# Three edits and a new step order in a fused attention, Fourier mixing and MLP kernel on one core

## The chip, the core and the metric

The kernel runs on one core of a Trainium2 chip. The metric is device time in microseconds for one launch. All inputs and the output lie in HBM; scratch tensors for intermediate tokens and for prepared weights lie there too.

## The reference

Chunked attention with memory keys feeds a Fourier mixing block with an MLP, and a gated convolutional MLP follows.

```python
# attention: batch 4, 8 heads, 768 tokens, head size 64; chunks of 32 queries
# look at 16 keys to the left, 8 to the right, and 8 memory keys
scores = scale * np.matmul(q_c, k_full.transpose(0, 1, 3, 2))
a = softmax(scores);  out[:, :, c_start:c_end] = np.matmul(a, v_full)
...
X = np.fft.fft(np.fft.fft(x, axis=1), axis=2)      # x: (4, 768, 512)
u = x + np.real(X)
un = (u - mu) / np.sqrt(var + 1e-06)
x = u + np.maximum(un @ w_ch1, 0.0) @ w_ch2        # 512 -> 2048 -> 512
...
h = np.maximum(x @ w_in, 0.0)                      # 512 -> 1024
gate = sigmoid(conv over 3 tokens of h)
return (h * gate) @ w_out                          # 1024 -> 512
```

## The kernel before

Every matrix product of the Fourier and MLP parts is made from three products of numbers split in a high and a low part (float32r): low by high, high by low, high by high. So each operand is prepared in two steps: ScalarE (ACT) copies the raw value into the high part, which rounds it, and VectorE (DVE) subtracts that from the raw value and writes the low part.

**Stage 1** handles attention and Fourier mixing, batch by batch (b = 0 to 3), in tiles of 128 tokens (t = 0 to 5). Its steps are named and put in order by hand in the table `ORDER`, one list for each of TensorE (PE), ACT, DVE and GpSimd (POOL); each engine takes its steps strictly in this order, and semaphores keep the data right. The steps on PE are `scores` (L507, q by the key window), `turn` (L517, transposes of the probabilities), `values` (L534), `seq` (L543, eight per batch, the transform over tokens), `dim` (L543, two per batch, the transform over channels) and `mix` (L599, transposes back). On ACT: `exp`, `keep` (copy of turned probabilities, L360), `split` (high part of folded tokens, L367), `bh` (L374), `qs` (L382), `mirror`. On DVE: `shift` (L421, L426), `norm` (L435 to L446), `bl` (L452), `cm` (L462, L463), `mk` (L473, L474, adds x and the mixed result). On POOL: `fold` (L315 to L321) and `lower` (L329, low part of folded tokens). `seq` of b needs the folded and lowered tokens; its first run also needs the table over tokens (`seq_tab`), the first `dim` the table over channels (`dim_tab`). Both tables come from HBM as ready high and low parts, issued by POOL's steps `tabs` and `tabd`, in the middle of the loads of q, k and v, which the DMA queue of SyncE (SP) issues in a ring of three tiles.

**Stage 2** is the first MLP, for each batch in two groups of four pairs. A pair n expands tokens by two 128-column blocks of `w_ch1` in seven products of six matmuls (L975, a Strassen-like scheme: seven weight blocks, of which three are loaded ones, called A11, A12, A22 and one, S1, is loaded and then changed, and S2, S3, S4 are sums). The preparation of a pair is: `load_raw1` (SP, two loads, L712 and L714), `sums` (POOL, four adds, L758 to L764), `weights1` (ACT L771 for all seven high parts, DVE L813 for all seven low parts), and `store_w1` (POOL's queue, L725), which keeps the finished pair in HBM for later batches. The weights lie in a ring of three buffers, so pair 3 takes the buffer of pair 0 and waits for its products and its store. Results of a pair pass through `keep_first` (ACT, L801), `combine` and `complete` (DVE, seven adds L890, and four low parts L894) and `rectify` (ACT, L806). After four pairs comes `contract` (L995), eight weight tiles loaded by `load_raw2` (SP, L721). For the first batch the banks of the contraction are those in which the pair's results stood, so token tile 3 of its first weight tile waits until `complete(3)` has made all its adds.

The first pairs are worked into stage 1 by steps called `mlp`: on PE `mlp0` to `mlp2` turn normalised tokens, `mlp3` and `mlp4` are pair 0 and `mlp5` and `mlp6` pair 1. SP puts the stores of the last batch's tokens (`store_u`, L268) between the load of pair 2 and that of pair 3.

**Stage 3** is the gated convolution (L1327, L1337).

Of the kernel before, what the change touches and what calls it, by code (L numbers as in the profile page):

```python
# [1599 lines left out]
```

## Time and profile before

| | us |
|---|---|
| median of 3 runs | 993.39 |
| lowest and highest | 991.74, 995.04 |
| the profiled execution, its time | 991.06 |
| the profiled execution, its span | 989.3 |
| PE busy | 943.7 |
| DVE busy | 624.9 |
| ACT busy | 346.7 |
| POOL busy | 221.1 |

The rows below are times from the start of the span. In a row of a timeline the first number is the start, the second the duration; the bracket at the end tells how long the engine had been idle and what ended the wait. L975 is line 975 of the kernel before.

### The profile page before, as it was taken

The page shows a single profiled execution, that of the slowest core. Times are in us where ns is not written, and L with a number is a line of the kernel's source. Part 1 is how long each engine was busy: PE and PEld are TensorE (multiplying, and loading weights), DVE is VectorE, ACT ScalarE, POOL GpSimd, SP SyncE. Part 2 cuts the span into 40 slices and gives each one's busy share as a digit, 9 for nine tenths or more (in the row PEclk, how much of TensorE's full clock was granted, in tenths as well). Part 3 has the DMA queues.
Part 4 walks back from the last instruction along what each step waited for, and adds up shares of the span by engine and source line. Part 5 has one row for each costly group of instructions (what it writes and reads, how often), then busy time and mean ns, then how long its engine had stood idle before and what let it go on. Part 6 is the DMA issues. An engine that isn't in the chain of part 4 may idle for free.

```text
span 989.3 us, 15359 instructions
## 1 busy us (share of the span) xinstructions
PE 943.7 (95%) x6168; PEld 850.1 (86%) x6168; DVE 624.9 (63%) x1034; ACT 346.7 (35%) x583; POOL 221.1 (22%) x231
## 2 busy tenths in 40 slices
PE   5899997859999999999999999999999999999998
PEld 4788786858897998989989889898898898998997
DVE  5467759658586773776827767266486295393590
ACT  2444555314244231332312323124253254253341
POOL 5757758114020000000000000000024033042041
PEclk9999999889999999999999999999999999999999
DMA  9956733567435672544824536355120300301001
GB/s 336 356 178 235 277 120 108 217 230 283 184 142 231 215 260 67 195 147 155 308 79 161 181 117 233 129 160 179 60 70 1 128 1 22 106 0 42 22 1 64
DMA packets 50033, 148.41 MB, mean 150 GB/s; under 512 B 7856, under 2 KB 12080, under 8 KB 45616
## 3 DMA queue, kind: packets, MB, share of 16 engines
q1 hardware_dynamic: 44640, 85.16, 25.0%
q0 software_dynamic: 5184, 62.27, 16.8%
q8 instruction: 46, 0.75, 0.3%
q14 instruction: 19, 0.16, 0.0%
q10 hardware_dynamic: 144, 0.07, 0.0%
HBM read 115.50 MB, written 31.98 MB: 149 GB/s over the span
## 4 chain that ended last, share of the span: by engine, by line
PE 85%; DVE 5%; DMA 4%; POOL 3%; issue 1%; SPq 1%; ACT 1%; DVEq 0%; POOLq 0%; ACTq 0%
PE ps L995 25%; PE ps L975 22%; PE ps L1327 13%; PE ps L1337 13%; PE ps L543 5%; DMA k_win<-in_k 2%; PE ps L507 2%; DMA w_raw<-in_moe_w 1%; PE ps L1310 1%; PE ps L534 1%; PE ps L936 1%; DVE h_raw L890 1%; DVE w L813 1%; PE ps L517 1%; DVE h L894 1%
## 5 line engine op out<-in xcount | busy, mean ns | idle before, releaser
L995 PE MATMUL ps<-w,h 128*128 128x512 f32 x1152 | 267.3, 391 | 0.4 <-DVE h_raw L890 0.4
L995 PEld LDWEIGHTS ps<-w,h 128*128 128x128 f32 x1152 | 215.0, 188 | 44.6 <-DVE h_raw L890 0.8
L975 PE MATMUL ps<-x_hi,w 128*128 128x384 f32 x896 | 232.8, 338 | 11.5 <-DVE w L813 10.1
L975 PEld LDWEIGHTS ps<-x_hi,w 128*128 128x128 f32 x896 | 164.2, 190 | 12.8 <-DVE w L813 10.7
L890 DVE TENSOR_TENSOR h_raw<-h_raw,ps 128x384 f32<-128x384 f32 x224 | 122.8, 552 | 59.6 <-PE ps L975 53.5
L975 PE MATMUL ps<-x_lo,w 128*128 128x384 f32 x448 | 151.1, 337 | 0.0
L1327 PE MATMUL ps<-y_hi,v 128*128 128x384 f32 x512 | 130.6, 334 | 0.0
L806 ACT ACTIVATE h<-h_raw 128x384 fp32r<-128x384 f32 x128 | 67.0, 526 | 157.0 <-DVE h_raw L890 154.9
L1337 PE MATMUL ps<-v,g_hi 128*128 128x512 f32 x384 | 118.9, 391 | 0.0
L1395 POOL TENSOR_TENSOR g_lo<-conv,g_hi 128x768 fp32r<-128x768 f32 x32 | 68.8, 2154 | 185.7 <-ACT g_hi L1258 185.7
L1289 DVE SCALAR_TENSOR_TENSOR conv<-h_pad,taps,conv 128x768 f32<-128x768 f32 x64 | 100.5, 1570 | 2.3
L1327 PEld LDWEIGHTS ps<-y_hi,v 128*128 128x128 f32 x512 | 92.5, 188 | 0.2
L734 POOL DMA_DIRECT2D w<-w_scratch x24 | 12.7, 531 | 355.6 <-PE ps L975 355.6
L1327 PE MATMUL ps<-y_lo,v 128*128 128x384 f32 x256 | 85.6, 334 | 0.0
L975 PEld LDWEIGHTS ps<-x_lo,w 128*128 128x128 f32 x448 | 85.1, 190 | 0.3
L1337 PEld LDWEIGHTS ps<-v,g_hi 128*128 128x128 f32 x384 | 72.2, 188 | 14.8
L818 DVE TENSOR_TENSOR w<-w_raw,w 128x512 fp32r<-128x512 f32 x64 | 44.3, 701 | 52.1 <-ACT w L775 52.1
L1337 PE MATMUL ps<-v,g_lo 128*128 128x512 f32 x192 | 76.5, 399 | 0.0
L894 DVE SCALAR_TENSOR_TENSOR h<-h_raw,h 128x384 fp32r<-128x384 f32 x128 | 67.7, 570 | 11.5 <-ACT h L806 11.5
L775 ACT ACTIVATE w<-w_raw 128x512 fp32r<-128x512 f32 x64 | 38.5, 626 | 70.8 <-DMA w_raw<-in_moe_w 70.8
L1277 DVE TENSOR_TENSOR y_lo<-ps,y_hi 128x512 fp32r<-128x512 f32 x24 | 16.5, 690 | 63.9 <-ACT y_hi L1239 63.9
L1327 PEld LDWEIGHTS ps<-y_lo,v 128*128 128x128 f32 x256 | 48.1, 188 | 0.1
(110 smaller groups left out, 1166.8 us busy)
## 6 DMA issues: line engine op xcount, KB each, us to landing
w<-w_scratch POOLq DMA_DIRECT2D x24, 1792.0 KB, 7.6
w_raw<-in_moe_w SPq DMA_DIRECT2D x80, 256.0 KB, 2.9
w_scratch<-w POOLq DMA_DIRECT2D x8, 1792.0 KB, 8.2
v_win<-in_v SPq DMA_DIRECT2D x48, 260.0 KB, 5.0
k_win<-in_k SPq DMA_DIRECT2D x48, 256.0 KB, 5.0
q_sb<-in_q SPq DMA_DIRECT2D x24, 256.0 KB, 4.6
y_scratch<-u SPq DMA_DIRECT2D x8, 768.0 KB, 4.6
y_in<-y_scratch SPq DMA_DIRECT2D x4, 1536.0 KB, 7.1
```

The lines of the kernel that those rows point to most:

```text
L543: last = nc.tensor.matmul(out, lhs, rhs, start=(n == 0), stop=(n == 3 * len(terms) - 1))
L775: nc.scalar.activation(w2[j % R2][:, 0], w2_raw[j % R2][:, 1], ACT.Copy).then_inc(w2_hi_ready, 1)
L806: nc.scalar.activation(hidden(m, half, 0), raw_hidden(m, half), ACT.Relu).then_inc(relu_done, 1)
L818: nc.vector.tensor_tensor(w2[j % R2][:, 1], w2_raw[j % R2][:, 1], raw(w2[j % R2][:, 0]), ALU.subtract).then_inc(w2_ready, 1)
L890: nc.vector.tensor_tensor(out, a, result(n, i), ALU.add).then_inc(summed, 1)
L894: nc.vector.scalar_tensor_tensor(out=hidden(m, half, 1), in0=raw_hidden(m, half), scalar=0.0, in1=raw(hidden(m, half, 0)), op0=ALU.max, op ...
L975: last = nc.tensor.matmul(result(n, i), a, b, start=(k == 0), stop=(k == 5))
L995: last = nc.tensor.matmul(ps[:, t, :], h[:, m, part, cols], w2[j % R2][:, weight], start=(m == 0 and i == 0), stop=(m == GROUP - 1 and i = ...
L1289: nc.vector.scalar_tensor_tensor(out=c, in0=h[:, j:S + j], scalar=taps[:, m, j:j + 1], in1=c, op0=ALU.mult, op1=ALU.add).then_inc(tap_done ...
L1327: last = nc.tensor.matmul(ps[:, BH[m % 2] + half, 0:HALF], w[:, cols], y[:, c, toks], start=(k == 0), stop=(k == 3 * ND - 1))
L1337: last = nc.tensor.matmul(ps[:, BACC[t], :], g[:, m, cols], w, start=(m == 0 and j == 0), stop=(m == M2T - 1 and j == 2))
L1395: nc.gpsimd.tensor_tensor(g_lo[:, m, :], conv[:, m % 3, :], g_hi[:, m, :].bitcast(F32), ALU.subtract).then_inc(g_lo_ready, 1)
```

## The change

Four things are changed.

1. `load_raw1(3)` moves on SP's queue ahead of the last batch's `store_u`, and `store_w1(0)`, which it waits for, moves from the start of stage 2 on POOL's queue to a place inside stage 1, ahead of the sums of pair 2.
2. The seven weight blocks are laid out anew, so that the three that are needed as loaded (`BLOCKS`) and the four that POOL changes or makes (`SUMS`) are contiguous, and `weights1` becomes `blocks1` and `sums1` on ACT and on DVE. ACT's `blocks1` waits only for the load.
3. The tables come from HBM in plain form; a new step on ACT (`tabhi`) rounds them and a new step on DVE (`tablo`) makes the low part.
4. `ORDER` is rewritten.

```diff
@@ sync, stage 1
                 if i == 0:
                     for j in range(FOLDS):
                         store_u(2, j)
+            mlp_sync(sp, FOLDS)
             for i in range(FOLDS):
                 store_u(B - 1, i)
@@ gpsimd, scalar, vector, stage 1
-                for dst, src in zip(pairs, (tables[0], tables[1])):
-                    pool.dma_start(dst[:], src).then_inc(landed, 16)
+            def load_table(i):
+                pool.wait_ge(scored, (2, 5)[i])
+                pool.dma_start((seq_raw, dim_raw)[i][:], (seq_tab, dim_tab)[i]).then_inc((ld_seq, ld_dim)[i], 16)
+            def upper_table(i):
+                act.wait_ge((ld_seq, ld_dim)[i], 16)
+                nc.scalar.activation((seq_hi, dim_hi)[i][:], (seq_raw, dim_raw)[i][:], ACT.Copy).then_inc(table_hi_ready, 1)
+            def lower_table(i):
+                dve.wait_ge(table_hi_ready, i + 1)
+                nc.vector.tensor_tensor((seq_lo, dim_lo)[i][:], (seq_raw, dim_raw)[i][:],
+                                        (seq_hi, dim_hi)[i][:].bitcast(F32), ALU.subtract).then_inc(table_ready, 1)
@@ stage 2
-    A11, S2, S1, S3, A12, S4, A22 = range(7)
+    S4, S3, S2, S1, A22, A11, A12 = range(7)
+    SUMS, BLOCKS = slice(S4, S1 + 1), slice(A22, A12 + 1)
...
-        def weights1(n):
+        def blocks1(n):
+            act.wait_ge(ld_raw1[n % 3], 32 * (n // 3 + 1))
+            nc.scalar.activation(w1[n % 3][:, BLOCKS, 0], w1_raw[n % 3][:, BLOCKS, 1], ACT.Copy).then_inc(a1_hi_ready, 1)
+        def sums1(n):
             act.wait_ge(s_ready, n + 1)
-            nc.scalar.activation(w1[n % 3][:, :, 0], w1_raw[n % 3][:, :, 1], ACT.Copy).then_inc(w1_hi_ready, 1)
+            nc.scalar.activation(w1[n % 3][:, SUMS, 0], w1_raw[n % 3][:, SUMS, 1], ACT.Copy).then_inc(s1_hi_ready, 1)
@@ scalar, stage 2
                     if n >= 2:
+                        early = 3 <= n + 1 < PAIRS and n + 1 not in (5, 6)
+                        if early:
+                            blocks1(n + 1)
                         keep_first(n)
-                        if 3 <= n + 1 < PAIRS and n + 1 not in (5, 6):
-                            weights1(n + 1)
+                        if early:
+                            sums1(n + 1)
                         rectify(n)
@@ vector, stage 2
                         combine(n)
-                            weights1(n + 1)
+                            blocks1(n + 1)
+                            sums1(n + 1)
                         complete(n)
@@ ORDER, tensor, around the first seq (one line of the table)
-        "scores0.4 turn0.3 values0.3 turn0.4 scores0.5 values0.4 scores1.0 turn0.5 values0.5 seq0.0 turn1.0 "
+        "values0.2 turn0.3 scores0.5 turn0.4 values0.3 scores1.0 turn0.5 values0.4 scores1.1 turn1.0 "
+        "values0.5 seq0.0 ..."
```

The order of instructions at three places. On ACT, at the start of the program (rows of one kernel carry other line numbers than those of the other; L353 and L345 are `exp`, L360 and L352 `keep`, L367 and L359 `split`). Before:

```order
L353 ACTIVATE probs<-probs 128x512
L367 ACTIVATE z_hi<-z_raw 128x4x128
L360 ACTIVATE p_sb<-ps 128x512
L353 ACTIVATE probs<-probs 128x512
L367 ACTIVATE z_hi<-z_raw 128x4x128
L360 ACTIVATE p_sb<-ps 128x512
L353 ACTIVATE probs<-probs 128x512
```

The same place on ACT in the changed kernel:

```order
L345 ACTIVATE probs<-probs 128x512
L359 ACTIVATE z_hi<-z_raw 128x4x128
L392 ACTIVATE seq_hi<-seq_lo_raw 128x2316
L352 ACTIVATE p_sb<-ps 128x512
L345 ACTIVATE probs<-probs 128x512
L359 ACTIVATE z_hi<-z_raw 128x4x128
L345 ACTIVATE probs<-probs 128x512
```

The rounding of the 2316 columns of the table over tokens now stands ahead of a `keep` and an `exp`.

On ACT, from the preparation of pair 2 (buffer w_2) to that of pair 4 (w_1). Before:

```order
L801 ACTIVATE h_raw<-ps 128x384
L771 ACTIVATE w_2_63<-w_2_raw 128x7x256
L382 ACTIVATE q_sin<-ps 128x386
L806 ACTIVATE h<-h_raw 128x384 x4
...
L801 ACTIVATE h_raw<-ps 128x384
L771 ACTIVATE w_0_59<-w_0_raw 128x7x256
L806 ACTIVATE h<-h_raw 128x384 x4
L775 ACTIVATE w_0_67<-w_0_raw 128x512
L775 ACTIVATE w_1_69<-w_1_raw 128x512
L801 ACTIVATE h_raw<-ps 128x384
L771 ACTIVATE w_1_61<-w_1_raw 128x7x256
```

The same stretch in the changed kernel (L779 is `blocks1`, L783 `sums1`, L813 `keep_first`, L818 `rectify`, L374 `qs`):

```order
L779 ACTIVATE w_2_63<-w_2_raw 128x3x256
L813 ACTIVATE h_raw<-ps 128x384
L374 ACTIVATE q_sin<-ps 128x386
L783 ACTIVATE w_2_63<-w_2_raw 128x4x256
L818 ACTIVATE h<-h_raw 128x384 x4
...
L818 ACTIVATE h<-h_raw 128x384 x4
L787 ACTIVATE w_0_67<-w_0_raw 128x512
L787 ACTIVATE w_1_69<-w_1_raw 128x512
L779 ACTIVATE w_1_61<-w_1_raw 128x3x256
L813 ACTIVATE h_raw<-ps 128x384
L783 ACTIVATE w_1_61<-w_1_raw 128x4x256
```

The part of the preparation that needs only the load now stands ahead of `keep_first`, and `qs` of the last batch stands ahead of the part that needs POOL's sums.

On SP, from the load of pair 2 on. Before (L268 is `store_u` of the last batch, L721 `load_raw2`):

```order
L712 DMA w_2_raw<-in_moe_w 128x2x256
L714 DMA w_2_raw<-in_moe_w 128x2x256
L268 DMA u_scratch<-x_odd 128x2x512 x3
L1050 UNCONDITIONAL_BRANCH
L712 DMA w_0_raw<-in_moe_w 128x2x256
L714 DMA w_0_raw<-in_moe_w 128x2x256
```

And in the changed kernel:

```order
L719 DMA w_2_raw<-in_moe_w 128x2x256
L721 DMA w_2_raw<-in_moe_w 128x2x256
L719 DMA w_0_raw<-in_moe_w 128x2x256
L721 DMA w_0_raw<-in_moe_w 128x2x256
L270 DMA u_scratch<-x_odd 128x2x512 x3
```

The load of pair 3 (buffer w_0) now stands ahead of the three stores; the seven `load_raw2` and then the load of pair 4 stand behind them, as before.

## Rows read from the trace of the kernel before

**Rows 1.** The page, busy time and share of each engine.

```profile
PE 943.7 (95%) x6168; PEld 850.1 (86%) x6168; DVE 624.9 (63%) x1034; ACT 346.7 (35%) x583; POOL 221.1 (22%) x231
```

**Rows 2.** Busy time in windows; at the end clock, DMA share, GB/s.

```profile
20.00:25.00 5.00, 2.39 (x64) 1.71 (x53) 3.30 (x8) 1.98 (x4) 3.82 (x5) 1.00 1.03 410
45.00:50.00 5.00, 5.00 (x35) 4.92 (x32) 2.93 (x5) 2.98 (x7) 1.88 (x2) 1.00 0.31 122
```

**Rows 3.** DMA issues of the first 50 us: size, median to landing.

```profile
seq_hi<-in_seq_tab POOLq DMA_DIRECT2D x1, 1158.0 KB, 9.3
dim_hi<-in_dim_tab POOLq DMA_DIRECT2D x1, 576.0 KB, 6.8
```

**Rows 4.** Timeline of PE, stage 1: the waits that matter.

```profile
25.59 1.93 PE L507 MATMUL ps<-k_win,q_sb 128*32 128x128 f32 x32 [2.46 <-DMA k_win<-in_k]
...
37.44 0.41 PE L543 MATMUL ps<-seq_hi,z_lo 128*128 128x386 f32 x1 [0.77 <-POOL z_lo L329]
...
116.46 1.08 PE L507 MATMUL ps<-k_win,q_sb 128*32 128x128 f32 x32 [1.53 <-DMA k_win<-in_k]
```

**Rows 5.** Timelines of ACT, DVE and POOL: single preparation steps.

```profile
171.44 1.70 ACT L771 ACTIVATE w<-w_raw 128x1792 fp32r<-128x1792 f32 x1 [2.83 <-POOL w_raw L764]
173.05 1.04 ACT L794 ACTIVATE x_hi<-x_lo_raw 128x1024 fp32r<-128x1024 f32 x1
...
166.32 2.01 DVE L813 TENSOR_TENSOR w<-w_raw,w 128x1792 fp32r<-128x1792 f32 x1
168.73 1.28 DVE L883 TENSOR_TENSOR x_lo<-x_lo_raw,x_hi 128x1024 fp32r<-128x1024 f32 x1
...
166.50 2.43 POOL L760 TENSOR_TENSOR w_raw<-w_raw 128x256 f32<-128x256 f32 x1
```

**Rows 6.** Windows again: the stretch before the first pairs.

```profile
148.40:173.10 24.70, 18.84 (x142) 17.10 (x141) 23.74 (x47) 14.31 (x28) 19.97 (x20) 0.98 0.31 108
```

**Rows 7.** Timelines of POOL, DVE, PE: pair 2 and last mixing.

```profile
182.64 0.73 POOL L758 TENSOR_TENSOR w_raw<-w_raw 128x256 f32<-128x256 f32 x1 [11.23 <-DMA w_raw<-in_moe_w]
...
188.38 0.56 DVE L894 SCALAR_TENSOR_TENSOR h<-h_raw,h 128x384 fp32r<-128x384 f32 x1 [3.41 <-ACT h L806]
...
191.87 2.31 PE L599 MATMUL ps<-ident_sb,m_all 128*128 128x128 f32 x12 [3.28 <-DVE m_all L463]
```

**Rows 8.** Timelines of SP, PE and POOL: pairs 2, 3 and contraction.

```profile
201.47 7.05 SPq L268 DMA_DIRECT2D u_scratch<-x_odd  x3
208.63 0.40 SPq L712 DMA_DIRECT2D w_raw<-in_moe_w  x1
...
213.70 0.59 SPq L712 DMA_DIRECT2D w_raw<-in_moe_w  x1
...
205.16 0.41 PE L975 MATMUL ps<-x_hi,w 128*128 128x384 f32 x1 [1.43 <-DVE h_raw L890]
221.81 0.69 PE L975 MATMUL ps<-x_hi,w 128*128 128x384 f32 x1 [9.13 <-DVE w L813]
...
234.02 6.19 PE L995 MATMUL ps<-w,h 128*128 128x512 f32 x26 [0.40 <-DVE h_raw L890]
...
213.97 0.72 POOL L758 TENSOR_TENSOR w_raw<-w_raw 128x256 f32<-128x256 f32 x1 [22.27 <-DMA w_raw<-in_moe_w]
```

**Rows 9.** Windows of 2 us after the long wait.

```profile
222.00:224.00 2.00, 2.00 (x7) 2.00 (x8) 1.97 (x5) 1.68 (x4) 1.85 (x3) 0.50 0.53 229
224.00:226.00 2.00, 2.00 (x8) 2.00 (x7) 2.00 (x3) 1.25 (x3) 1.84 (x3) 0.50 1.05 444
...
228.00:230.00 2.00, 2.00 (x14) 2.00 (x13) 1.56 (x5) 0.68 (x2) 0.00 (x0) 1.00 0.00 0
```

**Rows 10.** Weight loads issued from 213.0 to 215.7 us.

```profile
DMA to landing us min/median/max: 5.7/6.6/6.7
```

**Rows 11.** The page's group of adds, then PE's start of pair 7.

```profile
L890 DVE TENSOR_TENSOR h_raw<-h_raw,ps 128x384 f32<-128x384 f32 x224 | 122.8, 552 | 59.6 <-PE ps L975 53.5
...
287.76 0.45 PE L975 MATMUL ps<-x_hi,w 128*128 128x384 f32 x1 [0.97 <-DVE w L813]
```

More of the change, by code:

```diff
@@ L185, in attention_and_fourier @@
     seq_hi = sb("seq_hi", [P, 2, FOLDS, NF], F32R)
-    seq_lo = sb("seq_lo", [P, 2, FOLDS, NF], F32R)
+    seq_lo, seq_raw = sb.both("seq_lo", [P, 2, FOLDS, NF])
     dim_hi = sb("dim_hi", [P, 9, P], F32R)
-    dim_lo = sb("dim_lo", [P, 9, P], F32R)
+    dim_lo, dim_raw = sb.both("dim_lo", [P, 9, P])
     b_hi = sb("b_hi", [P, ND, 2, NF], F32R)
@@ L340, in _ @@
                     lower(b, t)
-                elif step == "tabs":
-                    load_seq()
-                elif step == "tabd":
-                    load_dim()
+                elif step == "table":
+                    load_table(t)
         @block.scalar
@@ L480, in _ @@
                     mlp_vector(dve, t)
+                elif step == "tablo":
+                    lower_table(t)
                 elif step == "shift":
@@ L655, in channel_mlp @@
     s_added, s_ready = sem("s_added"), sem("s_ready")
[L656 removed]
+    a1_hi_ready, a1_ready, s1_hi_ready, s1_ready = (sem(f"{name}_ready") for name in ("a1_hi", "a1", "s1_hi", "s1"))
     w2_hi_ready, w2_ready = sem("w2_hi_ready"), sem("w2_ready")
@@ L748, in first_sync @@
                 sp.wait_ge(core.st_u[j], 16 * 2)
-        else:
+        elif i == 2:
             sp.wait_ge(core.seq_done, 8 * B)
@@ L806, in rectify, with lower1, blocks1, sums1 @@
                 nc.scalar.activation(hidden(m, half, 0), raw_hidden(m, half), ACT.Relu).then_inc(relu_done, 1)
-        return weights1, weights2, square_root, upper, upper_sums, keep_first, rectify
+        return blocks1, sums1, weights2, square_root, upper, upper_sums, keep_first, rectify
     def on_vector(dve):
-        def weights1(n):
-            dve.wait_ge(w1_hi_ready, n + 1)
-            nc.vector.tensor_tensor(w1[n % 3][:, :, 1], w1_raw[n % 3][:, :, 1], raw(w1[n % 3][:, :, 0]), ALU.subtract
-                                    ).then_inc(w1_ready, 1)
+        def lower1(n, part, ready):
+            nc.vector.tensor_tensor(w1[n % 3][:, part, 1], w1_raw[n % 3][:, part, 1], raw(w1[n % 3][:, part, 0]),
+                                    ALU.subtract).then_inc(ready, 1)
+        def blocks1(n):
+            dve.wait_ge(a1_hi_ready, n + 1)
+            dve.wait_ge(s_ready, n + 1)
+            lower1(n, BLOCKS, a1_ready)
+        def sums1(n):
+            dve.wait_ge(s1_hi_ready, n + 1)
+            lower1(n, SUMS, s1_ready)
         def weights2(j):
@@ L921, in add_up @@
             nc.vector.tensor_tensor(u_sb[b % 2][:, t, :], ps[:, t, :], u_sb[b % 2][:, t, :], ALU.add).then_inc(y_ready, 1)
-        return (weights1, weights2, stats, variance, inverse_root, normalise, lower, lower_sums, combine, complete,
+        return (blocks1, sums1, weights2, stats, variance, inverse_root, normalise, lower, lower_sums, combine, complete,
                 add_up)
@@ L1004, in first_gpsimd @@
     def first_gpsimd(pool, k):
+        if k == 2:
+            store_w1(pool, 0)
         on_gpsimd(pool)(k)
     def first_scalar(act, k):
-        weights1, weights2, square_root, upper, upper_sums, keep_first, rectify = on_scalar(act)
+        blocks1, sums1, weights2, square_root, upper, upper_sums, keep_first, rectify = on_scalar(act)
         if k == 0:
@@ L1013, in first_scalar @@
         elif k < 10:
-            weights1(k - 7)
+            sums1(k - 7)
+        elif k > 13:
+            blocks1(k - 14)
         else:
@@ L1018, in first_vector @@
     def first_vector(dve, k):
-        (weights1, weights2, stats, variance, inverse_root, normalise, lower, lower_sums, combine, complete,
+        (blocks1, sums1, weights2, stats, variance, inverse_root, normalise, lower, lower_sums, combine, complete,
          add_up) = on_vector(dve)
@@ L1034, in first_vector @@
         elif k < 16:
-            weights1(k - 13)
+            sums1(k - 13)
+        elif k > 19:
+            blocks1(k - 20)
         else:
@@ L1082, in _ @@
             sums = on_gpsimd(pool)
-            for n in range(PAIRS):
+            for n in range(1, PAIRS):
                 store_w1(pool, n)
@@ L1093, in _ @@
         def _(act):
-            weights1, weights2, square_root, upper, upper_sums, keep_first, rectify = on_scalar(act)
+            blocks1, sums1, weights2, square_root, upper, upper_sums, keep_first, rectify = on_scalar(act)
             for g in range(2 * B):
@@ L1113, in _ @@
                     if g == 0 and m in (0, 3):
-                        weights1(5 + m // 3)
+                        blocks1(5 + m // 3)
+                        sums1(5 + m // 3)
                     if second and b + 1 < B and m in (1, 3, 5):
@@ L1123, in _ @@
         def _(dve):
-            (weights1, weights2, stats, variance, inverse_root, normalise, lower, lower_sums, combine, complete,
+            (blocks1, sums1, weights2, stats, variance, inverse_root, normalise, lower, lower_sums, combine, complete,
              add_up) = on_vector(dve)
@@ L1130, in _ @@
                     if n >= 2:
+                        early = 3 <= n + 1 < PAIRS and n + 1 not in (5, 6)
                         combine(n)
-                        if 3 <= n + 1 < PAIRS and n + 1 not in (5, 6):
-                            weights1(n + 1)
+                        if early:
+                            blocks1(n + 1)
+                            sums1(n + 1)
                         complete(n)
@@ L1146, in _ @@
                     if g == 0 and m in (0, 3):
-                        weights1(5 + m // 3)
+                        blocks1(5 + m // 3)
+                        sums1(5 + m // 3)
                     if not second and b + 1 < B and m < TILES:
@@ L1537, in constants @@
     mats.append(fix)
-    return {"seq_tab": halves(seq), "dim_tab": halves(np.stack(mats, axis=1)), "ident": np.eye(P, dtype=np.float32)}
+    return {"seq_tab": seq.astype(np.float32), "dim_tab": np.stack(mats, axis=1).astype(np.float32), "ident": np.eye(P, dtype=np.float32)}
 def windows(x, mem):
```

32 lines of the change are left out of this document (12 added, 20 removed), and 71 rows, old and new, of the table ORDER.

## The prediction

> **What bounds the kernel.** I read the page first: PE is busy 943.7 of 989.3 us [rows 1], so at most some 45 us of waits and what a low clock costs can be won, and everything that merely speeds another engine is worth nothing unless PE waits for it. Then PE's timeline, for the waits. They lie at three places. In the first 45 us the DMA engines are full (share 1.03, 410 GB/s) while PE works 2.39 of 5 us; by 45 to 50 us the DMA share is 0.31 and PE has no gap [rows 2]. From there to about 146 us PE hardly waits; the largest wait is 1.53 us for a key window [rows 4]. From 148 to 173 us DVE is busy 23.74 of 24.70 us and PE 18.84 [rows 6]. After it come three waits in series: 3.28 us for DVE's `cm3.1` ahead of the last mixing [rows 7], 1.43 us ahead of pair 2 and 9.13 us ahead of pair 3 [rows 8]. From pair 3 on PE is nearly always busy, so a microsecond won before it stays won.
>
> **The long wait.** SP stores the last tokens from 201.47 to 208.52 and only then issues the load of pair 3 at 208.63; POOL begins its sums at 213.97 and PE pair 3 at 221.81 [rows 8]. After it the clock is at 0.50, the 1.2 of the two levels 1.2 and 2.4 GHz, for over 4 us: 7 and 8 matmuls in 2 us against 14 later, 13 fewer at 2/14 us, 1.9 us lost [rows 9]. The contraction behind it waits 0.40 more [rows 8]. Together 9.13 + 1.9 + 0.40 = 11.4 us.
>
> In the changed kernel the load goes out when pair 0's products and its store are done. Pair 0 ends where PE fell idle ahead of the mixing, 191.87 - 3.28 = 188.6 [rows 7], 20 us before 208.63, so POOL's sums are over well before pair 2 ends. What is left is DVE's order: `combine(2)`, both low parts, `complete(2)`. Pair 7 has the same order today and waits 0.97 us [rows 11]. Two instructions in place of one cost another 0.15: 1792 columns take 2.01 and 1024 take 1.28, so 0.95 ns a column and 0.3 fixed, part of which overlaps [rows 5]. Pair 3 waits **1.1 us**, too short to cost the clock: pair 2, behind a wait of 1.43, took 7.5 us (worked out below), no more than a warm pair of 42 matmuls at 2/14 us and its gaps.
>
> **What is late next.** ACT now does `blocks1(4)` ahead of `keep_first(3)`, and `blocks1(4)` waits for the load of pair 4. That load still stands behind the stores and seven `load_raw2` on SP. Let S be the start of pair 2, 205.16 before. The last store's issue ends at S + 3.35 (208.52), the load of pair 4 goes at S + 8.5 (213.70) and loads of that moment land 5.7 to 6.7 us after issue [rows 8, 10]. Without the 512 KB of pair 3 in front (1.3 us at 410 GB/s) and with no change else, it lands at about S + 13.9. PE takes 221.81 - 9.13 - 205.16 = 7.5 us for a pair [rows 8], so pair 3 runs from S + 8.6 to S + 16.1, and token tile 3 of the contraction is due after nine matmuls of 6.19/26 = 0.24 us, at S + 18.2. But its bank is free only after `complete(3)`. From the start of the sums to PE's start of a pair takes 221.81 - 213.97 = 7.84 us today [rows 8], with one `rectify` and one low part in the chain; ACT's piece of 1024 columns in place of 1792 takes 1.04 against 1.70 [rows 5], DVE's two pieces 0.15 more, three adds of 0.55 follow [rows 11]: 7.84 - 0.66 + 0.15 + 1.65 = 9.0. The bank is free at S + 13.9 + 9.0 = S + 22.9, so PE waits **4.7 us** in the contraction, and by the 3.28 us of [rows 7], after which twelve transposes took 2.31 us, the clock falls again; I take the same 1.9. Queued behind the load in ACT are `keep_first(3)`, then `rectify(3)`; DVE's `combine(3)` waits for the first, PE for DVE. Today the same chain is hidden by the 9.13 us. So of 11.4 us 1.1 + 4.7 + 1.9 = 7.7 stay: **gain 3.7**. Bounds: the load could land up to 2 us later or up to 5 earlier, if the queue is emptier than today's; so 1.5 to 10.3 (no wait and no cold clock).
>
> **Ahead of the last mixing.** After the last `seq` PE does pair 0 and `dim3.1`, until 188.6. Sums of pair 2 start at 182.64, ACT then does all seven blocks, and DVE's low part waits 3.41 us for ACT's `rectify`, until 188.38; then L813 (2.02) and `cm3.1` follow [rows 7]. In the new order `cm3.1` stands directly behind that low part, but `qs3.1` stands ahead of `sums1(2)`, and `qs3.1` needs `dim3.1`, which ends 2.1 us (twelve matmuls of 0.17) before 188.6, so at 186.5. Then `qs` 0.5, `sums1` 1.04, `rectify` 0.5, low part 0.55, `cm3.1` 1.1: 190.2 against 191.87. **Gain 1.6**; up to 3.3 if PE does not wait, none if ACT is held up at `blocks1(2)`, whose load also stands ahead of `keep_first(0)`.
>
> **The stretch on DVE.** From 148 us to `cm3.0` DVE is full, so its list is the length [rows 6]. The list is nearly the same; one `norm` of about 1.1 us falls ahead of the stretch and two splits add 0.3. **Gain 0.8**, between -1 and 2, as PE's turns and `seq` steps come in another order and could leave a gap on DVE.
>
> **Tables.** The loads shrink by one of each pair, 1158 + 576 = 1734 KB [rows 3], 4.2 us at 410 GB/s: the upper bound. Against it stand the new steps, ahead of work on the first tiles. The first half of the table over tokens lands 9.3 us after issue today [rows 3], and it is the raw table now; issued behind `scores0.1`, that is at about 21.5. ACT then rounds 2316 columns, by [rows 5] 1.70 + 524 x 0.86 ns = 2.15 us, with `keep0.2` and `exp0.3` queued behind it; DVE subtracts in 2.5 us with `norm0.2` behind it. The window of `scores0.4`, 25.59 today [rows 4], lands 1158 KB or 2.8 us sooner. DVE has it shifted by about 25.3, `tablo` ends at 27.9, `norm0.2` at 29.0; POOL then folds tiles 2 and 3 (four adds of 0.72, 2.9 us each) and lowers tile 2 (about 1.3): 36.1, against 37.44 for `seq0.0` [rows 4]. `scores1.1` and `turn1.0`, 1.6 us of PE, now lie ahead of it, which moves work into idle time. The table over channels adds 1.15 on ACT and 1.4 on DVE, hidden behind the keys that still arrive. That makes 1.3 + 1.6 = 2.9, less what tile 7's keys cost (by the same rate they come at 33.5, so `values0.5` ends at 36.5, not 36.1) and less what POOL loses to DVE. A POOL add of 0.72 us took 2.43 while DVE's L813, a subtraction of two SBUF operands, ran beside it [rows 5, 8], 1.7 lost. DVE's 1.4 us for the second table falls into POOL's fold of tile 3, and I charge 1.1. **Gain 1.4**, from -3 (both subtractions and ACT's rounding in the chain) to 4.2.
> The Trainium skill, SBUF — State Buffer, section "SBUF: two separate sides", states an exclusive lock: a DVE operation with two SBUF inputs and a GpSimd operation that reads SBUF block each other for a whole instruction. By that rule the tables' subtractions, which this change adds, speak against it: up to 1.4 us for the second and a share of the first, and the sum would be smaller by some 0.3 to 1. The trace agrees with it in the one row named.
>
> **Key windows and the middle.** PE has no gaps to win there but the 1.53 us of [rows 4] and smaller ones; the new order may keep or lose it. **Gain 0.5**, 0 to 1.5.
>
> **Sum.** 3.7 + 1.6 + 0.8 + 1.4 + 0.5 = 8.0. The profiled execution took 991.06 (span 989.3), which is 2.3 under the median, so it would become 983.1 and the median 993.39 - 8.0 = **985.4**.
>
> **Rivals.**
> 1. *The load of pair 4 is in time.* Then the contraction does not wait and the clock stays: 6.6 more, 978.8. For it: SP's queue may run ahead once the stores are out, and the load has product and store conditions that are long met. Against it: landing would have to be 5 us sooner, while seven loads and 1.8 MB are in front. Chance 0.22 (range 975 to 982).
> 2. *The tables pay in full*, 4.2 instead of 1.4, contraction as forecast: 982.6. For it: DMA at 1.03; against: ACT and DVE in the chain. Chance 0.13.
> 3. *No change.* The edits only hand the waits on: tables -3, DVE's stretch -1, the mixing 0, pair 3 1.5 or so; 990.4 to 996. Chance 0.10.
> 4. *Slower.* SP now waits inside stage 1 for `store_w1(0)` to land, with the last three stores, all `load_raw2` and the load of pair 4 queued behind. If that store came late, all of them and the contraction would slip with it, one for one. It would have to delay the load of pair 4 by 8.0 us to cancel the gain and by 11 to show, landing at S + 25. It is issued ahead of the sums of pair 2 (182.64) and 1792 KB take 4.4 us at 410 GB/s, so it is done 10 us early. Past that point: 997 to 1002. Chance 0.05.
> The forecast itself: 0.50, its own range 982 to 989.
>
> **Range and chances.** From rival 1's middle to the edge of no change: 977 to 990.5. A measurement of this kernel tells about 0.3% (3 us) from no change: faster means under 990.4. Faster 0.50 + 0.22 + 0.13 = 0.85, same 0.10, slower 0.05.
>
> **What would show it.** Right: the load of pair 3 issued before the last stores; PE's wait ahead of pair 3 near 1.1 us at full clock; a new wait of 3 to 6 us inside the first nine matmuls of L995, behind DVE's adds, with ACT idle for a DMA at `blocks1(4)` ahead of `keep_first(3)`; the last mixing about 1.6 us nearer to the last `seq`; the first `seq` at about 36.5 with `scores1.1` ahead of it. Wrong: no wait in the contraction (rival 1), a first `seq` after 38 (ACT or DVE late with the table), a gap on DVE between 148 and 173, or new waits of PE between 50 and 146 us.

## The result and the profile after

The changed kernel takes **985.93 us** (median of five, 985.29 to 987.12); the kernel before took 993.76 beside it (five, 991.74 to 995.04). The ratio is 0.9926, 95% interval 0.9915 to 0.9938. That is 7.8 us faster by the medians and 7.4 us (0.74%) by the ratio, against 985.4 and 8.0 forecast. The profiled execution of the changed kernel took 985.29 (span 983.5), that of before 991.06 (span 989.3), so the pair of traces shows only 5.8 us; the traced execution of before was a quick one. Run 2 below has the step order and the tables of before, and its trace (993.12) comes to the last mixing at 193.39, where that of before comes at 191.87: 1.5 us of such spread lie ahead of that point. Of run 10 below one execution took 1688.5 us at a granted clock of 0.749 against 0.988 to 0.993 in its others, and is left out of every number.

The page of the changed kernel, as in [rows 1], and PE's waits by cause (total, how many, longest):

```profile
PE 942.5 (96%) x6168; PEld 850.2 (86%) x6168; DVE 629.7 (64%) x1044; ACT 351.9 (36%) x593; POOL 218.5 (22%) x229
```

```profile
PE ps L513 <- DMA k_win<-in_k: 12.1, 5, 6.1
PE ps L1017 <- DVE h_raw L911: 3.8, 1, 3.8
PE ps L540 <- DVE x_even L444: 3.8, 2, 3.5
PE ps L549 <- DVE b_lo L450: 3.4, 2, 3.2
```

The 9.13 us ahead of pair 3 are gone from the list and 3.8 us of a contraction (L1017) are new. PE's timeline of the changed kernel at the places of [rows 4, 7, 8, 11] (start, duration, in brackets the wait and who ended it):

```profile
22.64 1.93 PE L513 MATMUL ps<-k_win,q_sb 128*32 128x128 f32 x32 [4.26 <-DMA k_win<-in_k]
...
31.64 1.36 PE L540 MATMUL ps<-v_win,p_sb 128*32 128x130 f32 x32 [3.47 <-DVE x_even L444]
...
40.11 0.41 PE L549 MATMUL ps<-seq_hi,z_lo 128*128 128x386 f32 x1 [0.40 <-POOL z_lo L323]
...
190.75 1.53 PE L605 MATMUL ps<-ident_sb,m_all 128*128 128x128 f32 x12 [1.38 <-DVE m_all L461]
...
202.89 0.56 PE L997 MATMUL ps<-x_hi,w 128*128 128x384 f32 x1 [1.89 <-DVE h_raw L911]
...
213.08 0.41 PE L997 MATMUL ps<-x_hi,w 128*128 128x384 f32 x1 [1.08 <-issue]
...
220.44 2.25 PE L1017 MATMUL ps<-w,h 128*128 128x512 f32 x9
226.52 3.07 PE L1017 MATMUL ps<-w,h 128*128 128x512 f32 x7 [3.83 <-DVE h_raw L911]
...
282.00 0.41 PE L997 MATMUL ps<-x_hi,w 128*128 128x384 f32 x1 [1.08 <-issue]
```

Read as milestones against [rows 4, 7, 8, 11]: the first `seq` 2.7 us later with 1.6 us of other work now ahead of it, the last mixing 1.12 earlier, pair 2 2.27 earlier, pair 3 8.73 earlier, the contraction 7.5 earlier and pair 7 5.76 earlier. What pair 3 won is partly given back twice, in the new wait of 3.83 and in the low clock behind it: from the end of the contraction's wait to pair 7 it was 53.74 us before and is 55.48 now. SP, ACT and POOL of the changed kernel show who holds the contraction:

```profile
189.41 0.37 SPq L719 DMA_DIRECT2D w_raw<-in_moe_w  x1
...
198.77 7.49 SPq L270 DMA_DIRECT2D u_scratch<-x_odd  x3
206.30 3.78 SPq L728 DMA_DIRECT2D w_raw<-in_moe_w  x7
210.19 0.41 SPq L719 DMA_DIRECT2D w_raw<-in_moe_w  x1
210.64 0.66 SPq L721 DMA_DIRECT2D w_raw<-in_moe_w  x1
```

```profile
217.61 0.84 ACT L779 ACTIVATE w<-w_raw 128x768 fp32r<-128x768 f32 x1 [1.51 <-DMA w_raw<-in_moe_w]
218.36 0.47 ACT L813 ACTIVATE h_raw<-ps 128x384 f32<-128x384 f32 x1
220.88 1.06 ACT L783 ACTIVATE w<-w_raw 128x1024 fp32r<-128x1024 f32 x1 [2.05 <-POOL w_raw L772]
221.85 0.51 ACT L818 ACTIVATE h<-h_raw 128x384 fp32r<-128x384 f32 x1
```

```profile
213.52 0.57 POOL L733 DMA_DIRECT2D w_scratch<-w  x1 [12.31 <-DVE w L824]
217.67 0.73 POOL L766 TENSOR_TENSOR w_raw<-w_raw 128x256 f32<-128x256 f32 x1 [3.58 <-DMA w_raw<-in_moe_w]
```

The load of pair 3 (189.41) is 9 us ahead of the stores. That of pair 4 goes out at 210.19, behind stores and seven loads, and lands at 217.6. ACT has by then waited 1.51 us at `blocks1(4)`, with `keep_first(3)` (L813) behind it; it waits again for POOL's sums at `sums1(4)`, with `rectify(3)` (L818) behind that.

The clock, windows as in [rows 9] (the third number from the end is the granted clock, 0.50 being 1.2 and 1.00 being 2.4 GHz), after the wait ahead of pair 2 and after the one in the contraction:

```profile
204.00:206.00 2.00, 2.00 (x8) 2.00 (x7) 1.87 (x5) 2.00 (x4) 0.00 (x0) 0.50 0.82 312
...
228.00:230.00 2.00, 2.00 (x6) 1.54 (x6) 2.00 (x3) 1.42 (x4) 1.78 (x2) 0.50 0.81 182
```

### The profile page after: what moved, and what is told of

It reads as the page before. It is cut to its first block, busy times and chain, and to the rows that moved or that the text cites. A ratio compares the mean times of both kernels' runs of the same rounds, so it can differ in the third digit from the quotient of the medians.

```text
span 983.5 us, 15393 instructions
## 1 busy us (share of the span) xinstructions
PE 942.5 (96%) x6168; PEld 850.2 (86%) x6168; DVE 629.7 (64%) x1044; ACT 351.9 (36%) x593; POOL 218.5 (22%) x229
## 4 chain that ended last, share of the span: by engine, by line
PE 85%; DVE 6%; DMA 3%; POOL 2%; SPq 2%; issue 2%; ACT 0%; DVEq 0%; POOLq 0%; ACTq 0%
PE ps L1017 25%; PE ps L997 22%; PE ps L1362 14%; PE ps L1372 13%; PE ps L549 5%; DMA k_win<-in_k 2%; PE ps L513 1%; PE ps L540 1%; PE ps L1345 1%; PE ps L957 1%; DMA u_scratch<-x_odd 1%; DMA w_raw<-in_moe_w 1%; SPq L265 1%; DVE h_raw L911 1%; PE ps L605 1%
## 5 line engine op out<-in xcount | busy, mean ns | idle before, releaser
L1017 PE MATMUL ps<-w,h 128*128 128x512 f32 x1152 | 268.9, 393 | 3.8 <-DVE h_raw L911 3.8
L1017 PEld LDWEIGHTS ps<-w,h 128*128 128x128 f32 x1152 | 216.1, 189 | 48.6 <-DVE h_raw L911 4.3
L818 ACT ACTIVATE h<-h_raw 128x384 fp32r<-128x384 f32 x128 | 67.0, 526 | 157.6 <-DVE h_raw L911 155.7
L942 DVE TENSOR_TENSOR u<-ps,u 128x512 f32<-128x512 f32 x48 | 32.3, 690 | 25.4 <-PE ps L1017 25.4
```

The lines of the kernel that those rows point to most:

```text
L818: nc.scalar.activation(hidden(m, half, 0), raw_hidden(m, half), ACT.Relu).then_inc(relu_done, 1)
L1017: last = nc.tensor.matmul(ps[:, t, :], h[:, m, part, cols], w2[j % R2][:, weight], start=(m == 0 and i == 0), stop=(m == GROUP - 1 and i = ...
```

## The experiments

Ten kernels; each is compared with the kernel before, run beside it on the same chip. The kernel before has the median 992.96 beside runs 1 to 4, 993.79 beside runs 5, 6, 7 and 9, and 993.09 beside runs 8 and 10, so two runs of different groups are best compared by their ratios.

**1. Pair 4 last.** Is the contraction's wait due to pair 4's preparation standing ahead of `rectify(3)` and `complete(3)`?

```diff
-                        early = 3 <= n + 1 < PAIRS and n + 1 not in (5, 6)
+                        early = 3 <= n + 1 < PAIRS and n + 1 not in (4, 5, 6)
...
                         rectify(n)
+                        if n == 3:
+                            blocks1(4)
+                            sums1(4)
```

(on DVE the same behind `complete(3)`)

> The changed kernel, with the preparation of pair 4 (blocks1(4), sums1(4)) moved behind rectify(3) on ACT and behind complete(3) on DVE. Theory: the 3.83 us wait in the contraction comes from pair 4's late load standing in the chain keep_first(3), combine(3), rectify(3), complete(3); with it out of the chain the wait falls under 0.5 us, no slow clock follows (1.8 us), and the time is 5.6 us under the changed kernel, about 980.3. Rival: the wait is DVE's own load of work (seven adds, four low parts); then it stays near 3 us and the time near 985.

Measured **980.78** (980.24 to 980.94), ratio 0.9877 (0.9861 to 0.9894). PE has no wait in the contraction. The new wait and the clock behind it are worth 5 us (4.9 by the ratios), and the cause is the order on ACT and DVE.

**2. The early load alone**, on the kernel before (edit 1, nothing else).

```diff
+            mlp_sync(sp, FOLDS)
             for i in range(FOLDS):
                 store_u(B - 1, i)
...
+        if k == 2:
+            store_w1(pool, 0)
```

> The kernel before, with edit 1 alone (load of pair 3 ahead of the last stores, store of pair 0 inside stage 1), old order, unsplit weights, ready tables. Theory: the early load alone gives nearly all that pair 3 gives: its wait falls from 9.13 to about 1 us, a new wait of 3 to 4.5 us comes in the contraction because weights1(4) stands in the chain there too; net 3.5 us under the kernel before, about 990.2. Rival: the split of the weights is what makes it possible, and without it pair 3 waits 2 us or more and the contraction 5 or more; then under 2 us are gained.

Measured **993.03** (988.48 to 996.88, twelve executions), ratio 1.0000 (0.9986 to 1.0014): a miss by 2.8 us, and the most telling run. PE's timeline of this kernel:

```profile
206.66 0.41 PE L976 MATMUL ps<-x_hi,w 128*128 128x384 f32 x1 [1.43 <-DVE h_raw L891]
215.15 0.44 PE L976 MATMUL ps<-x_hi,w 128*128 128x384 f32 x1 [0.97 <-DVE w L814]
234.72 1.65 PE L996 MATMUL ps<-w,h 128*128 128x512 f32 x3 [9.91 <-DVE h_raw L891]
```

and its POOL:

```profile
225.37 0.71 POOL L759 TENSOR_TENSOR w_raw<-w_raw 128x256 f32<-128x256 f32 x1 [9.40 <-DMA w_raw<-in_moe_w]
```

The wait ahead of pair 3 falls from 9.13 to 0.97, as forecast for this edit, and comes back whole, 9.91 us, one stage later, where I had expected 3 to 4.5. Pair 4's load, issued at 213.95, landed only at 225.37, 11.4 us later. Moving a load cleared one wait and the next one of the same chain took its place. The contraction's wait ends 9.35 us behind this landing, against 8.9 in the changed kernel, so the split of the weights saves about 0.5 us there; most of the difference between the two waits (9.91 and 3.83) is the later landing.

**3. `keep_first(3)` ahead of `blocks1(4)`** on ACT: it takes away the first of ACT's two waits for pair 4 and leaves the second.

```diff
-                        if early:
+                        if early and n != 3:
                             blocks1(n + 1)
                         keep_first(n)
+                        if early and n == 3:
+                            blocks1(n + 1)
```

> The changed kernel, with keep_first(3) put ahead of blocks1(4) on ACT and nothing else moved; sums1(4) stays ahead of rectify(3), and DVE's order is untouched. Theory: what binds is POOL's sums, then sums1(4), rectify(3) and the low part; the contraction's wait stays at 3.5 to 4 us and the time at 985.9. Rival: keep_first(3), held until 218.4 by blocks1(4), is what binds; then the wait falls by about 3 us and the time to about 982.

Measured **987.44** (983.09 to 989.8), ratio 0.9938 (0.9916 to 0.996); no gain. The contraction waits 8.95 us in its trace, because the load of pair 4 takes 11.1 us to land and not 7.4. ACT's timeline of this kernel:

```profile
213.52 0.47 ACT L813 ACTIVATE h_raw<-ps 128x384 f32<-128x384 f32 x1
220.31 0.84 ACT L779 ACTIVATE w<-w_raw 128x768 fp32r<-128x768 f32 x1 [6.32 <-DMA w_raw<-in_moe_w]
223.52 1.06 ACT L783 ACTIVATE w<-w_raw 128x1024 fp32r<-128x1024 f32 x1 [2.36 <-POOL w_raw L772]
224.48 0.51 ACT L818 ACTIVATE h<-h_raw 128x384 fp32r<-128x384 f32 x1
```

`keep_first` is done at 214 and of no use; `rectify(3)` still follows the sums. The contraction's wait ends at 229.15, 8.9 us behind the landing (220.3), as it ended 8.9 behind 217.6 in the changed kernel.

**4. The tables' steps later** (`tabhi0.0` behind `exp0.3`, `tablo0.0` behind `norm0.3`).

```diff
-        "exp0.0 keep0.0 exp0.1 keep0.1 exp0.2 split0.0 tabhi0.0 keep0.2 exp0.3 split0.1 exp0.4 keep0.3 "
+        "exp0.0 keep0.0 exp0.1 keep0.1 exp0.2 split0.0 keep0.2 exp0.3 tabhi0.0 split0.1 exp0.4 keep0.3 "
...
-        "shift0.0 shift0.1 norm0.0 shift0.2 norm0.1 shift0.3 shift0.4 tablo0.0 norm0.2 shift0.5 norm0.3 "
+        "shift0.0 shift0.1 norm0.0 shift0.2 norm0.1 shift0.3 shift0.4 norm0.2 shift0.5 norm0.3 tablo0.0 "
```

> The changed kernel, with the table over tokens rounded on ACT behind exp0.3 and subtracted on DVE behind norm0.3 instead of ahead of norm0.2. Theory: the 4.49 us subtraction ahead of norm0.2 holds values0.3 up by 3.47 us; placed later it costs PE nothing, the first seq starts at 37 to 38 instead of 40.1, and the time is 2 to 2.5 us under the changed kernel, about 983.5. Rival: the keys' and values' loads set the pace up to 45 us anyway; then the first seq starts earlier but PE waits for loads afterwards, and the time is within 1 us of 985.9.

Measured **983.58** (982.74 to 989.13), ratio 0.9915 (0.9893 to 0.9937). The first `seq` starts at 38.94 instead of 40.11, so the step did hold the first tiles up; by the ratios the gain over the changed kernel is not resolved, and the contraction's waits (3.45 and 3.97 us in its trace) would take what comes early.

**5. Ready tables** (on the kernel of 1, edit 3 undone: both halves loaded, no rounding or subtraction on the chip).

```diff
-                pool.dma_start((seq_raw, dim_raw)[i][:], (seq_tab, dim_tab)[i]).then_inc((ld_seq, ld_dim)[i], 16)
+                for dst, src in zip(((seq_hi, seq_lo), (dim_hi, dim_lo))[i], (tab[0], tab[1])):
+                    pool.dma_start(dst[:], src).then_inc((ld_seq, ld_dim)[i], 16)
```

> The kernel of the run that moves pair 4's preparation (980.8 us), with edit 3 undone: both tables come as ready high and low parts, no table steps on ACT and DVE. Theory: edit 3 costs more on DVE and in PE's wait for values0.3 (2.95 to 3.47 us) than its 1734 KB save; the first seq starts at 38 to 39 instead of 40.7 and the time is about 979. Rival: the loads set the pace of the first 45 us; then 1734 KB at 410 GB/s come back as 2 to 4 us, about 984.

Measured **982.49** (981.07 to 983.17), ratio 0.9884 (0.9867 to 0.99), against 980.78 and 0.9877 (0.9861 to 0.9894) of run 1: edit 3 saves 1.7 us by the medians and 0.7 by the ratios, and as the intervals overlap this is not told apart from nothing. My theory that it cost 1.8 us is not borne out. The first `seq` of this trace starts only at 44.73, against 40.72 in that of run 1. PE waits for keys where the changed kernel waits for DVE:

```profile
26.45 1.94 PE L501 MATMUL ps<-k_win,q_sb 128*32 128x128 f32 x32 [4.85 <-DMA k_win<-in_k]
...
39.92 1.93 PE L501 MATMUL ps<-k_win,q_sb 128*32 128x128 f32 x32 [3.22 <-DMA k_win<-in_k]
```

The second of these is `scores1.1`, which only the new order has ahead of the first `seq`. In the old order it is the other way round: the first `seq` starts at 37.44 (before) and 38.05 (run 2) with ready tables and at 39.73 (run 6) with plain ones. By these traces edit 3 pays at this place only together with edit 4.

**6. The old order** (on the kernel of 1, the four lists of `ORDER` as before with only the table and split steps put in).

> The kernel of the run that moves pair 4's preparation (980.8 us), with the order of the kernel before; the table steps and the split weight steps are put at the nearest old places (each blocks1 right ahead of its sums1). Theory: of the new order the middle (1.5 us), the mixing (1.9) and the clock behind it (1.2) gain and the stretch on DVE loses 1.2; so the old order is 3 us slower, about 984. Rival: the order as such is worth nothing and the edits carry the gain; within 1 us of 980.8.

Measured **984.67** (983.77 to 985.31), ratio 0.9907 (0.9891 to 0.9924): with plain tables the new order is worth 3.9 us by the medians and 3.0 by the ratios. In its trace the last mixing waits 2.94 us and its twelve transposes take 2.60, near the 3.28 and 2.31 of before [rows 7].

```profile
196.05 2.60 PE L604 MATMUL ps<-ident_sb,m_all 128*128 128x128 f32 x12 [2.94 <-DVE m_all L460]
```

**7. Pair 3's store later** (POOL's `store_w1(3)` behind `sums(4)`).

```diff
             for n in range(1, PAIRS):
+                if n == 3:
+                    sums(4)
                 store_w1(pool, n)
-                if n >= 2 and n + 1 < PAIRS:
+                if n >= 2 and n != 3 and n + 1 < PAIRS:
                     sums(n + 1)
```

> The changed kernel, with the store of pair 3 (1792 KB, POOL's queue) put behind the sums of pair 4. Theory: that store shares the DMA engines with pair 4's load and holds it up by up to 4.4 us; landing took 7.4 us from issue where the store went out 3.3 us after the load, and 11 us where it went out 1.4 to 1.8 us after. With the store behind, landing takes 5.5 to 7 us, the contraction waits under 3.5 us, and the time is 983 to 985 with a spread under 2 us. Rival: the seven loads ahead set the landing; then nothing changes, 985.9.

Measured **984.7** (982.65 to 987.81), ratio 0.9908 (0.9879 to 0.9938), not told apart from the changed kernel. The load, issued at 211.75, lands at 218.1, 6.4 us later, as expected; but the contraction still waits 4.31 us, until 227.01, and the executions still lie 5 us apart. I had expected a wait under 3.5 us and executions within 2 us of each other.

**8. Pair 4's load first** (on SP, ahead of the seven `load_raw2`).

> The changed kernel with the load of pair 4 issued ahead of the seven loads of contraction weights on SP instead of behind them; nothing is left out. The load then goes out at about 206.3 us, where the first of the seven went (206.30), instead of 210.2. By the theory that the contraction's wait is the landing of pair 4 plus 8.9 us, with a landing 6.4 to 7.4 us after issue as in two runs so far, it lands at 212.7 to 213.7 and the bank is free at 221.6 to 222.6, against 222.7 at which PE comes there: no wait, no low clock behind it, and 3.8 + 0.9 us less: about 981, as with the order on ACT and DVE turned round (980.78). Rival: it is not the place in SP's queue that sets the landing but the traffic of the 1792 KB store of pair 3 and what is on the engines, so it lands 11 us after issue, at 217, the wait stays 3 us or more, and the time is 984 to 986. A second rival: the seven loads behind it come late and PE waits for the first contraction weights instead, 983 or more.

Measured **981.95** (980.86 to 985.05), ratio 0.9896 (0.9869 to 0.9924), 3 to 4 us faster than the changed kernel, though the two intervals still overlap a little. The time is near the forecast, but a wait of 2.41 us stays (until 224.91) where I had expected none. The load goes out at 206.17; POOL's `store_w1(3)` stands ahead of the sums, so these start at 213.93, and now DVE holds the chain, with no gap from 210 to 224.9. DVE and POOL of this kernel:

```profile
214.23 2.91 DVE L915 SCALAR_TENSOR_TENSOR h<-h_raw,h 128x384 fp32r<-128x384 f32 x3
217.06 1.82 DVE L839 TENSOR_TENSOR w<-w_raw,w 128x512 fp32r<-128x512 f32 x2
```

```profile
214.76 0.95 POOL L768 TENSOR_TENSOR w_raw<-w_raw 128x256 f32<-128x256 f32 x1
```

In the changed kernel the same DVE groups took 1.49 and 1.29 with POOL idle, and POOL's add 0.74. The 1.95 us that DVE loses to POOL's four adds are most of the wait that is left.

**9. Runs 1 and 4 together.**

> Both moves together: pair 4's preparation behind rectify(3) and complete(3), and the table over tokens rounded and subtracted later. Theory: the two add up; first seq at about 39, no wait in the contraction, 978.8. Rival: what the tables give back is lost to later waits for keys and values; 980 to 981.

Measured **977.81** (975.62 to 979.41), ratio 0.9847 (0.9829 to 0.9864), the fastest of all and 3.0 us under run 1 by medians and ratios. Its first `seq` starts at 38.98 against 40.72 there. With no wait left in the contraction, the early microseconds of run 4 arrive at the end.

**10. Three `mlp` steps back to their old places**, on the kernel of 9 (`mlp1` on PE behind `seq3.1`, `mlp3` on ACT behind `bh3.0`, `mlp9` on DVE behind `bl3.0`).

> The kernel with pair 4's parts last and the tables' steps later (977.81), and in addition three steps put where the old order had them around the last batch: mlp1 on PE behind seq3.1 instead of ahead of seq3.0, mlp3 on ACT behind bh3.0, mlp9 on DVE behind bl3.0; nothing is left out. In the profile of the changed kernel DVE idles 0.80, 0.73 and 1.32 us between 148 and 177 us, and the last seq ends 1.2 us later after its start than before. Theory: these gaps come from the places of the mlp steps, which make PE's seq 3.0 and ACT's qs come later; undone, the stretch is 1.0 to 1.2 us shorter: about 976.7. Rival: the gaps come from the turns' and the splits' new places and not from these three, or DVE's list is full anyway: no change, 977.8, or up to 1 us slower because pair 0's turned tokens are made later.

Measured 980.59 (median of three, 980.35 to 983.29), ratio 0.9875 (0.985 to 0.99). That is 2.8 us slower than run 9 by medians and ratios, with intervals that just overlap, where I had forecast 1.1 us faster. In the traces it takes 48.3 us from the mixing of batch 2 to the last mixing (146.20 to 194.48) against 43.1 in the kernel of 9 (145.20 to 188.31). PE of this kernel:

```profile
154.91 0.66 PE L549 MATMUL ps<-seq_hi,z_lo 128*128 128x386 f32 x1 [2.73 <-POOL z_lo L323]
...
165.66 1.06 PE L957 MATMUL ps<-ident_sb,un 128*128 128x128 f32 x8 [1.23 <-DVE x_lo L897]
...
174.09 0.69 PE L549 MATMUL ps<-b_hi,dim_lo 128*128 128x386 f32 x1 [4.21 <-DVE b_lo L450]
```

As I read the first row, `mlp1` ahead of `seq3.0` filled time in which PE would have waited for POOL's lowered tokens anyway.

## Why the prediction came out as it did

The time was right to 0.5 us, and that is luck in part. Of the five terms two were right to 0.3 us in the pair of traces, pair 3 with the contraction and the mixing, together 5.3 of the 8.0 us forecast. The other three (DVE's stretch, the tables, the middle), forecast at 2.7 us together, do not show. All three lie ahead of the load of pair 2. It goes out at 179.21 in the trace of before and at 180.42 in that of run 2, and at 179.05 to 181.57 in the five traces whose first stage is that of the changed kernel (its own and runs 1, 3, 7 and 8), on average 0.5 us later and not 2.7 earlier. Two things that I had not counted make up for them: 1.15 us behind the last mixing, and that most executions of before are slower than the traced one.

**Pair 3 and the contraction: forecast 3.7, in the traces 3.5.** Pair 3's wait was put at 1.1 and is 1.08. The new wait in the contraction was forecast at its place, behind the named steps, at 4.7 and is 3.83; the clock behind it at 1.9 and is 1.7 (55.48 - 53.74). The chain "landing plus 9.0 us" measures 8.9 in the changed kernel and in runs 3, 4 and 7. Two inputs were off and offset each other. The load lands at S + 14.7, not S + 13.9: it goes out 1.2 us sooner than I had it but takes 7.4, not 5.4. And pair 2 takes 9.1 us in this trace, not 7.5, because the wait of 1.89 us ahead of it (before: 1.43) was followed by the 1.2 GHz level; so PE comes to the contraction 1.6 us later. The step that failed is that I left pair 2 as it was, at 1.43 us of wait and 7.5 us; "too short to cost the clock" held for pair 3's 1.08. The wait grew because the low part at the end of `combine(1)`, which stands on DVE ahead of the adds of `complete(1)` that PE waits for, takes 0.98 us now. DVE before, and DVE and POOL of the changed kernel:

```profile
203.34 0.55 DVE L894 SCALAR_TENSOR_TENSOR h<-h_raw,h 128x384 fp32r<-128x384 f32 x1
```

```profile
200.64 0.98 DVE L915 SCALAR_TENSOR_TENSOR h<-h_raw,h 128x384 fp32r<-128x384 f32 x1
200.48 0.73 POOL L772 TENSOR_TENSOR w_raw<-w_raw 128x256 f32<-128x256 f32 x1
```

The add is the last of pair 3's sums, which edit 1 brought here. All nine traces with the new order have 0.98 to 1.00 for this low part and a wait of 1.88 to 1.91; runs 2 and 6, which have the early load and the old order, have POOL idle there, 0.55, and waits of 1.43 and 1.45.

How much of this term is left depends on the landing, which no row of before could give. Run 4 has the code of the changed kernel from pair 2 on. In its trace the load took 10.9 us, and from pair 2 to pair 7 it is 82.52 us, against 79.11 in the changed kernel and 82.60 before [rows 8, 11]. So the 3.5 us are what one execution shows, and another shows 0.1.

**That this wait decides the rest** is shown: without it (run 1) 5 us less; with the load earlier (run 8) 3 to 4 less; with the load's move alone (run 2), where the wait is 9.91, no gain at all. Rival 1, "the load of pair 4 is in time", needed a landing 5 us sooner than S + 13.9; it was 0.8 later.

**Ahead of the last mixing: forecast 1.6, measured 1.9.** From the end of the last `seq` (SP's load of pair 2, 179.21 before and 179.98 after) to the mixing it was 12.66 us and is 10.77, the wait 1.38 for 3.28. Not counted was that a shorter wait keeps the clock: the twelve transposes take 1.53, not the 2.31 of [rows 7], and pair 2 comes another 1.15 us nearer. Run 6 shows both together: with the old order 2.94 and 2.60.

**The stretch on DVE: forecast a gain of 0.8, in the pair of traces a loss of 1.2**, outside my -1 to 2. It is measured from the mixing of batch 2 to the load of pair 2, 31.54 us before and 32.71 now. The old order takes 32.51 in run 2 and 32.85 in run 6, though, and the new one 31.9 to 33.2 in runs 1, 3, 4, 5, 7, 8 and 9: the loss is not told apart from the spread, and the gain is not there either. In both old traces PE waits for a low part late in the stretch, 3.38 us until 170.53 before and 3.75 until 171.16 in run 2; from 170 to 172 the granted clock is 0.99 in the one and 0.50 in the other. "DVE is full, so its list is the length" is the step that failed. DVE has three gaps in the changed kernel where it was full before [rows 6]:

```profile
157.29 1.42 DVE L878 TENSOR_SCALAR un<-u,mv,root 128x512 f32<-128x512 f32 x2 [0.80 <-PE ps L957]
...
160.11 0.56 DVE L450 TENSOR_TENSOR b_lo<-ps,b_hi 128x386 fp32r<-128x386 f32 x1 [0.73 <-ACT b_hi L366]
...
177.01 0.56 DVE L460 TENSOR_TENSOR m_all<-ps,q_sin 128x385 f32<-128x385 f32 x1 [1.32 <-ACT q_sin L374]
```

I named a gap between 148 and 173 us as what would show this term wrong. The cause of the gaps isn't settled: run 10 tried the three steps that I suspected, and it got worse.

**Tables: forecast 1.4, in the pair of traces a loss of 1.1 at the first `seq`.** It starts 2.7 us later with 1.6 us more work ahead of it. The forecast took edits 3 and 4 together, and run 5, with its 0.7 to 1.7 us, asks only what edit 3 is worth within the new order, so it does not bear the 1.4 out. The first `seq` was to start at 36.5 and starts at 40.11, past the 38 that I had named as a sign of being wrong. DVE of the changed kernel:

```profile
25.97 4.49 DVE L478 TENSOR_TENSOR seq_lo<-seq_lo_raw,seq_hi 128x2316 fp32r<-128x2316 f32 x1
...
36.08 1.35 DVE L478 TENSOR_TENSOR dim_lo<-dim_lo_raw,dim_hi 128x1152 fp32r<-128x1152 f32 x1
```

and POOL at the same time:

```profile
25.50 2.52 POOL L323 TENSOR_TENSOR z_lo<-z_raw,z_hi 128x512 fp32r<-128x512 f32 x2
...
36.16 1.87 POOL L314 TENSOR_TENSOR z_raw<-sums 128x256 f32<-128x256 f32 x1
```

POOL's two subtractions run at their usual 1.26 each, until 28.02; DVE's ends at 30.46, 2.44 us after that. So the 2.5 us that I gave it were right, and 2.0 us of standing behind POOL were missing; it also starts 0.7 us later than I had it. In the second pair DVE came first, by 0.08 us: it takes its 1.35, and POOL's add ends 0.6 after it, 1.13 us late, as charged (1.1). This is the exclusive lock of the Trainium skill, SBUF — State Buffer, section "SBUF: two separate sides". I had applied it only against POOL, from the one row where POOL was the loser; the section says that whoever starts first holds the ports, and these four rows agree. In the new order ready tables would not be quicker, as PE waits for keys instead (run 5). Moved behind `norm0.3` the plain tables save 3.0 us in run 9 beside run 1. Rival 2, the tables paid in full at 4.2 and a time of 982.6, did not come.

**Key windows and the middle: forecast 0.5, in the pair of traces 1.5.** The wait of 1.53 at 116.46 [rows 4] is 0.74, and one of 0.78 is gone. But the mixing of batch 2 starts anywhere from 146.49 to 149.16 us in the five traces with the same first stage, and at 147.67 and 147.91 before and in run 2, so a term of this size can't be read from one pair.

**Sum.** In the pair of traces +1.1 for the first `seq` (tables and order together), -1.5, +1.2, -1.9, -1.15 and -3.5 give 5.8 us gained. The medians show 7.8. Rival 3 ("the edits only hand the waits on") is what happened to edit 1 alone. Rival 4, the early store, did not occur: the load of pair 3 went out at 189.41 with nothing waiting behind it.

## What to carry to other kernels

When a load is moved forward, follow the ring to the next load behind it in the same queue, and look at what stands behind its consumer in program order: here the early load alone was worth nothing (run 2), and putting the next pair's preparation behind `rectify` and `complete` was worth another 5 us (run 1). A wait that is left on the path also swallows gains made before it, so it is to be removed first (the move of run 4 gained 1 us by the ratios on the changed kernel, unresolved, and 3 us on top of run 1). Before a term of 1 or 2 us is read from a pair of traces, look how far several traces of the same code lie apart at that place: here up to 2.7 us. Of two engines that block each other, ask in both directions who starts first.
